# Sparse attention and a rational MLP on one core: another way in for the first two batches

## The reference

```
# 8 batches, 8 heads, 576 tokens, head size 64; q, k, v float32
scores = q @ k.T / 8
rel = pos[:, None] - pos[None, :]
mask_local   = (rel >= 0) & (rel < 32)                            # heads 0 to 3
mask_strided = (rel >= 0) & (pos[None, :] % 32 == pos[:, None] % 32)  # heads 4 to 7
attn = softmax(where(mask, scores, -1e9))
x = (attn @ v), heads side by side               # [4608, 512]
h = x @ w_in                                     # [4608, 2048]
P = a0 + a1*h + a2*h**2 + a3*h**3
Q = 1 + |b0|*|h| + |b1|*h**2
out = (P / (Q + 1e-6)) @ w_out                   # [4608, 512], float32
```

## Time and profile before

| | |
|---|---|
| median of 3 runs | 422.16 us (420.53 to 424.83) |
| the profiled execution | 421.72 us |
| its span, first to last instruction | 419.9 us |
| busy in the span: TensorE, VectorE, ScalarE | 330.4, 318.9, 323.1 us |
| DMA: moved, mean | 50.12 MB, 119 GB/s |
| share of the 16 DMA engines: q1 (SyncE's), q0 (POOL's) | 41.3%, 23.9% |

### The profile page before, as it was taken

How to read it: one execution, slowest core, us unless ns; L and a number is a source line. 1 busy time by engine, 2 the same in 40 slices (tenths; PEclk the granted TensorE clock), 3 DMA queues, 4 the chain that set the end, 5 groups by cost and what they waited for, 6 DMA issues and landing times.

```text
span 419.9 us, 10298 instructions
## 1 busy us (share of the span) xinstructions
PE 330.4 (79%) x4674; PEld 160.4 (38%) x4674; DVE 318.9 (76%) x266; ACT 323.1 (77%) x351; POOL 43.7 (10%) x70
## 2 busy tenths in 40 slices
PE   0104207979959998999799899999999999992995
PEld 0003105434424543444344444445444444440442
DVE  5002025488699769999589799988998998999992
ACT  0102015479897899999689899799999999999983
POOL 8000200204000050005006000230000000000000
PEclk9999999979988999999999999999999999997999
DMA  8999969958016959928988997499821000000232
GB/s 134 213 203 207 213 144 188 154 116 143 4 35 81 213 91 183 212 73 141 194 161 177 167 133 118 108 161 120 186 66 30 2 25 27 25 25 2 75 125 100
DMA packets 102899, 50.12 MB, mean 119 GB/s; under 512 B 90280, under 2 KB 95336, under 8 KB 102312
## 3 DMA queue, kind: packets, MB, share of 16 engines
q1 hardware_dynamic: 93576, 32.29, 41.3%
q0 software_dynamic: 9280, 17.18, 23.9%
HBM read 39.76 MB, written 19.46 MB: 141 GB/s over the span
## 4 chain that ended last, share of the span: by engine, by line
ACT 42%; PE 25%; DVE 11%; SPq 11%; DMA 7%; issue 4%; ACTq 0%
PE ps L833 12%; ACT z L784 10%; ACT u L798 9%; ACT h L768 9%; ACT u L803 9%; PE ps L764 8%; SPq L382 4%; SPq L392 4%; DVE u L794 4%; DMA out_dram<-os 3%; DMA ptL<-pL 2%; DVE u L791 2%; ACT os L841 2%; DMA z<-in_v_dram 2%; SPq L294 1%
## 5 line engine op out<-in xcount | busy, mean ns | idle before, releaser
L833 PE MATMUL ps<-Wout,h 128*128 128x512 bf16 x576 | 138.9, 387 | 8.6 <-DVE h L818 7.5
L764 PE MATMUL ps<-XT,Win 128*128 128x512 bf16 x576 | 137.6, 385 | 5.1 <-ACT h L768 2.6
L768 ACT ACTIVATE h<-ps 128x512 bf16<-128x512 f32 x144 | 84.0, 673 | 11.4 <-PE ps L764 10.9
L833 PEld LDWEIGHTS ps<-Wout,h 128*128 128x128 bf16 x576 | 54.6, 99 | 73.9 <-DVE h L818 8.4
L764 PEld LDWEIGHTS ps<-XT,Win 128*128 128x128 bf16 x576 | 54.2, 99 | 73.8 <-ACT h L768 8.2
L798 ACT ACTIVATE u<-u,consts 128x2048 bf16<-128x2048 bf16 (+1 forms) x40 | 74.2, 1903 | 4.8 <-DVE u L794 4.8
L803 ACT ACTIVATE u<-u 128x2048 bf16<-128x2048 bf16 (+1 forms) x40 | 72.1, 1817 | 0.1
L784 ACT ACTIVATE z<-h 128x2048 bf16<-128x2048 bf16 (+1 forms) x38 | 69.4, 1871 | 0.2
L818 DVE TENSOR_TENSOR h<-z,u 128x4096 bf16<-128x4096 bf16 (+2 forms) x21 | 41.6, 1980 | 2.4 <-ACT u L803 1.8
L794 DVE TENSOR_TENSOR u<-u,z 128x4096 bf16<-128x4096 bf16 (+2 forms) x21 | 41.6, 1982 | 0.4
L814 DVE TENSOR_TENSOR z<-z,h 128x4096 bf16<-128x4096 bf16 (+2 forms) x21 | 41.5, 1977 | 0.3
(11 more groups left out here) (79 smaller groups left out, 227.4 us busy)
## 6 DMA issues: line engine op xcount, KB each, us to landing
out_dram<-os SPq DMA_DIRECT2D x36, 256.0 KB, 2.5
qk<-in_k_dram POOLq DMA_DIRECT2D x14, 288.0 KB, 6.5
qk<-in_q_dram POOLq DMA_DIRECT2D x14, 288.0 KB, 7.7
Win<-in_moe_w_in_dram POOLq DMA_DIRECT2D x2, 1024.0 KB, 30.5
Wout<-in_moe_w_out_dram POOLq DMA_DIRECT2D x2, 1024.0 KB, 31.6
v<-in_v_dram POOLq DMA_DIRECT2D x6, 288.0 KB, 8.8
vL<-v SPq DMA_DIRECT2D x24, 72.0 KB, 3.7
vS<-in_v_dram POOLq DMA_DIRECT2D x24, 72.0 KB, 6.9
```

The costliest lines, as they stand in the source:

```text
L764: r = e.matmul(bank(ph, 0, CH), Win[:, kk, f * 128:(f + 1) * 128], XT[:, kk, c * CH:c * CH + CH], start=(kk == 0), stop=(kk == NK1 - 1))
L768: P.op("act", lambda e, f=f, ph=ph, h=h, f0=f0: e.activation(h.t[:, f - f0, :], bank(ph, 0, CH), AF.Copy), "ev512", ("hev", c, f), r=[ph], ...
L833: r = e.matmul(bank(po, 0, Fout), h.t[:, j, m * 128:(m + 1) * 128], Wout[:, kk, :], start=(kk == 0), stop=(kk == NF - 1))
```

## The change

- The constants go first in SyncE's queue, in the order IDN, MS, M0, each mask with a tile of its own (T_ms, T_m0); the masks' matmuls now also wait for the turned q and k that they go before.
- q and k of batches 0 and 1 are cast straight into SBUF, by pairs of heads (eight DMAs a batch, local heads first), and turned by TensorE. Batch 1's strided pairs are staged in Wout's second half, whose load waits for their turns.
- For these two batches the strided V is cast by POOL straight into vS, as for the others. The local V comes as float32, its own blocks only, by SyncE and, for half of batch 0, by ScalarE; both halves are cast by VectorE and ScalarE, and VectorE makes the copy one block up by two copies across partitions (vshift). Batch 1's loads wait for the last strided k of batch 0.
- Weights: Win's halves and Wout's first half stand between the casts of batches 0 and 1, Wout's second behind those of batch 2.
- Ln takes its bias as a number. The argument `dma=` changed its form; it tells the planner what a transfer costs and makes no instruction.
- `ORDER` and `AT` are new throughout.

```
-    NQK, NP = 1, 2
+    NQK, NP = 2, 2
...
-            for i, (nm, s_t, h0) in enumerate((("qs", q, HL), ("ks", k, HL), ("ql", q, 0), ("kl", k, 0))):
...
+            for i, (nm, s_t, h0) in enumerate((("ql", q, 0), ("kl", k, 0), ("qs", q, HL), ("ks", k, HL))):
+                for pair in range(2):
+                    if b != 1:
+                        ap = XT[0:72, i, NT - 2048 + 1024 * pair:NT - 1024 + 1024 * pair]
+                    elif i < 2:
+                        ap = XT[0:72, 2 * i + pair, 1536:2560]
+                    else:
+                        ap = Wout[0:72, 4 * i + 2 * pair:4 * i + 2 * pair + 2, :].rearrange("p h c -> p (h c)")
+                    t = Tile(f"sg{b}{nm}{pair}", ap.rearrange("p (h c) -> p h c", h=2))
+                    if b == 2:
+                        t.prev = stage[0, nm, pair].w + stage[0, nm, pair].r
+                    if b == 1 and i >= 2:
+                        T_wout[1].over.append(t)
+                    else:
+                        early.append(t)
+                    stage[b, nm, pair] = t
+                    P.op("pool", lambda e, t=t, s_t=s_t, h=h0 + 2 * pair: e.dma_start(
+                        t.t, bass.AP(tensor=s_t.tensor, offset=rows(s_t, b, h),
+                                     ap=[[8 * D, 72], [S * D, 2], [1, 8 * D]])),
+                        "issue", ("cast", b, nm), w=[t], dma=(144, 97), after=after)
...
-        if b < 2:
-            return st
-        bulk(b, "v", v, 0, vs, b * HS, T_v[b], after)
...
     def early_v(b, st):
 
+        vgate = [x for p in range(2) for x in stage[0, "ks", p].w]
...
+            for hh in range(2):
+                P.op("act" if b == 0 and hh else "sp", lambda e, hh=hh, pair=pair, t=t: e.dma_start(
+                    t.t[64 * hh + 32:64 * hh + 64, 0:NB * 64].rearrange("p (m d) -> p m d", d=64),
+                    bass.AP(tensor=v.tensor, offset=rows(v, b, 2 * pair + hh),
+                            ap=[[D, 32], [LB * D, NB], [1, D]])),
+                    "issue", ("vf", b, pair), w=[t], dma=(576, 21), after=vgate if b else ())
+            for hh in range(2):
+                e_ = ("dve", "act")[hh]
+                P.op(e_, evict(e_, lambda hh=hh, pair=pair: vl.t[64 * hh + 32:64 * hh + 64, pair, :, 0:64],
+                               lambda hh=hh, t=t: t.t[64 * hh + 32:64 * hh + 64, 0:NB * 64].rearrange(
+                                   "p (m d) -> p m d", d=64)), "cast1152", ("vcast", b, pair), r=[t], w=[vl])
+        own = list(vl.w)
+        for hh in range(2):
+            P.op("dve", lambda e, hh=hh: e.tensor_copy(
+                vl.t[64 * hh:64 * hh + 32, :, 1:NB, :], vl.t[64 * hh + 32:64 * hh + 64, :, 0:NB - 1, :]),
+                "cp2210", ("vshift", b), w=[vl], after=own)
 
...
-        P.op("pe", smask, "smask", ("smask", b), r=[T_c, T_id], w=[SS])
+        P.op("pe", smask, "smask", ("smask", b), r=[T_ms, T_id, sqk], w=[SS])
...
-        P.op("pe", lmask, "lmask", ("lmask", b), r=[T_c, T_id], w=[SL])
+        P.op("pe", lmask, "lmask", ("lmask", b), r=[T_m0, T_id, lqt, lkt], w=[SL])
...
-    for i in range(2):
-        weights(i, Wout[:, 8 * i:8 * i + 8, :], w_out[1024 * i:1024 * i + 1024, :], T_wout, "wout")
     sts[1] = casts(1)
     loads(0, sts[0])
+    weights(0, Wout[:, 0:8, :], w_out[0:1024, :], T_wout, "wout")
     nxt = 0
     for b in range(B):
         if b + 1 < B:
             loads(b + 1, sts[b + 1])
+        if b == 0:
+            weights(1, Wout[:, 8:16, :], w_out[1024:2048, :], T_wout, "wout")
...
-        "27 25 82 29 95 31 35 33 83 39 37 84 236 96-98 86 100 93 105 103 91 113 107 114 109 108 249 119 110 "
+        "39 41 43 45 47 106-109 49 51 53 111 93-95 116 114 97 124-125 104 102 66 128 130 118-121 70 68 72 147 "
```

More of the change, by code:

```diff
@@ L248, in graph @@
     T_wout = [Tile(f"wout{i}") for i in range(2)]
+    for t in T_win + T_wout:
+        t.over = []
     XT = sb("XT", [128, NK1, NT])
@@ L322, in bulk @@
             bass.AP(tensor=s_t.tensor, offset=rows(s_t, b, h0), ap=[[n, 16], [1, n]])),
-            "issue", ("cast", b, nm), w=[t], dma=1.5, after=after)
+            "issue", ("cast", b, nm), w=[t], dma=(16, 1380), after=after)
     stage = {}
@@ L354, in casts, with weights @@
                         ap=[[32 * D, NI], [S * D, HL], [1, 8 * D]])),
-                "issue", ("cast", b, "vS"), w=[vS], dma=0.45, after=after)
+                "issue", ("cast", b, "vS"), w=[vS], dma=(72, 97), after=after)
         return st
-    def weights(i, into, src, T, nm):
-        T[i].new()
+    def weights(i, into, src, T, nm, after=()):
+        T[i].new(*T[i].over)
         P.op("pool", lambda e: e.dma_start(into, src.rearrange("(a p) n -> p a n", p=128)), "issue", (nm, i),
-             w=[T[i]], dma=5.9)
+             w=[T[i]], dma=(512, 172), after=after)
@@ L373, in early_v @@
             t.new()
             host.over = [t]
-            fs.append(t)
-        for pair in range(2):
-            t = fs[pair]
-            P.op("dve", lambda e, t=t: e.memset(t.t[:, 0:64], 0.0), "tiny", ("vfz", b, pair), m=[t])
-            t.new()
-            for sh in range(2):
-                for hh in range(2):
-                    P.op("sp", lambda e, hh=hh, pair=pair, sh=sh, t=t: e.dma_start(
-                        t.t[64 * hh + 32 - 32 * sh:64 * hh + 64 - 32 * sh, 64 * sh:NB * 64].rearrange(
-                            "p (m d) -> p m d", d=64),
-                        bass.AP(tensor=v.tensor, offset=rows(v, b, 2 * pair + hh),
-                                ap=[[D, 32], [LB * D, NB - sh], [1, D]])),
-                        "issue", ("vf", b, pair), w=[t], dma=0.9)
@@ L388, in early_v @@
-        t = fs[2]
-        P.op("dve", lambda e, t=t: e.memset(t.t[:, 0:2048], 0.0), "mset", ("vfz", b, 2), m=[t])
-        t.new()
-        for bq in range(4):
-            P.op("sp", lambda e, bq=bq, t=t: e.dma_start(
-                t.t[32 * bq:32 * bq + NI, 0:2048].rearrange("p (h c) -> p h c", h=HL),
-                bass.AP(tensor=v.tensor, offset=rows(v, b, HL) + 8 * bq * D,
-                        ap=[[32 * D, NI], [S * D, HL], [1, 8 * D]])),
-                "issue", ("vfs", b), w=[t], dma=0.4)
@@ L444, in loads @@
                             ap=[[D, 32], [LB * D, NB], [1, D]])),
-                    "issue", ("load", b, "vl"), r=[T_v[b]], w=[own], dma=1.0)
+                    "issue", ("load", b, "vl"), r=[T_v[b]], w=[own], dma=(576, 16))
         for hh in range(2):
@@ L458, in turn_qk @@
         n = 0
-        for nm, dst in (("qs", sqk), ("ks", sqk), ("ql", lq), ("kl", lk)):
-            src = stage[b, nm]
+        for nm, dst in (("ql", lq), ("kl", lk), ("qs", sqk), ("ks", sqk)):
             for pair in range(2):
+                src = stage[b, nm, pair]
                 e_ = ("dve", "act")[pair]
```

89 lines of the change are left out of this document (32 added, 57 removed), and 103 rows, old and new, of the table ORDER.

## The result

| | before | after |
|---|---|---|
| median, us | 423.50 (420.53 to 425.10, 4 runs) | 375.84 (372.78 to 377.38, 4 runs) |
| ratio | 1 | 0.8873 [0.8793, 0.8953] |
| span of the profiled execution, us | 419.9 | 373.6 |
| first matmul of w1, us | 75.42 | 40.45 |
| from there to the end, us | 344.5 | 333.15 |

The time fell by 47.7 us, some 11%; 382 us was forecast, 365 to 398 the range. Inside that sum two terms were off, in opposite directions: the first part ended 8 us later than forecast (40.45 for 32), and the second was 15 us shorter (333.15 for 348.1).

The account below looks back on a forecast made before the run. Data was taken to bound the first part, compute (ScalarE and TensorE) the second. First w1 at 32 plus 348 made a 380 us span; 1.8 and 0.4 us more gave 382, range 365 to 398.

Parts of the forecast that it names:

- The bound: Whole kernel: up to 75.4 us it waits for data with DMA engines full; the other 344.5 us wait for compute.
- The landing: First part, batch 0's loads: the last k pair lands between 13 and 15.5 us, 14 taken.
- the upper value: Batch 0's loads: 15.5 us for q and k if POOL's, SyncE's and ScalarE's queues take three turns, V landing with them.
- So the last k pair lands ..., 3.3 us, so 17.3: Batch 0's attention: transposes, eviction, strided mask and scores take 3.3 us from last k pair to maximum, at 17.3.
- From the maximum to the first w1: End of first part: 14.6 us as before, plus shifts 1.6 and turns 1.8, less masks 1.7 and local maximum 1.35.
- The second part: From first w1 to the end: 344.5 us as before plus 3.6 of ScalarE's added work, 348.1; new order at nothing.
- priced at nothing: Ln's bias as a number: takes away one more thing to load, no time counted.
- the second part tightens: Rival, second part: the new order removes two DMA waits and ScalarE's idling, some 12 us, total 370; chance 0.11.
- V last: Rival, first part: ScalarE's and SyncE's loads share one queue, V holds the attention, w1 at 38, 388 us; chance 0.13.
- Batch 2 last: Rival: batch 2's casts stand behind 6.1 MB; with slower DMAs TensorE waits some 10 us, 392 us; chance 0.09.
- The clock: Rival, second part: TensorE at 1.2 GHz for part of its matmuls gives back some or all gain, 425 us; chance 0.05.
- the band of the forecast itself: Whole time: start moved by 43 us, second part as before and 4 us more, 372 to 391 us; chance 0.62.

Follow-up runs that it names:

- the first w1 at 35.70: Changed kernel with batch 1's three turns ahead of the first w1 put behind the first four groups of w1; 375.60 us, ratio 0.8903.
- the second of the V runs: Kernel before with batch 0's V ahead of batch 1's on SyncE's queue and batch 1's V casts behind batch 0's attention; 419.08 us, ratio 0.9906.

## Why the prediction was right, and where two terms were not

- **The bound.** "The first part waits for data, the second for compute": borne out. The gain is 35 us in front and 11 behind.
- **The landing.** The last k pair had landed by 15.44, when SyncE's load that waits for it was issued: inside the 13 to 15.5 given, above the 14 taken. The three queues that were the condition of the upper value are there, but not its three turns: ScalarE's queue had moved 1093 of its 1184 packets by 3.5 us, when POOL's had moved one, and the rest by 6.25. That the upper value came out is luck; what held the last pair beyond 14 us is not shown.
- **The step that was short: "So the last k pair lands ..., 3.3 us, so 17.3".** The maximum came at 21.05. On TensorE the local mask, scores and negation (1.03 + 1.24 + 1.14 = 3.4 us) stand ahead of the strided turns and scores, so that the chain ran through them and not from the last landing; and a fetch took 0.50.
- **From the maximum to the first w1** 14.95 us were forecast and 19.4 measured. 6.67 of these are program fetches (0.66 + 2.24 + 3.77), a wait that the sum did not have; without them the stretch was 12.7, 2 us under the forecast, which was not taken apart. In all: 32.3 + 3.75 + 6.67 - 2.2 = 40.5. The trace of before had shown such a stall: 3.3 us of "issue" stand in front of the strided scores in the very row used for their duration, hidden there behind the wait for V.
- **The second part.** 348.1 forecast; less 3.8 of ScalarE's work, most of it Ln ("priced at nothing"), and 11.15 of its idle time: 333.15. The rival "the second part tightens" was right on the waits and their size (11 for "some 12"), and it was given 0.11; its total, 370 us, stood on a first w1 at 32.
- **"V last", "Batch 2 last", the clock.** The first fell with one queue. The second did not come about, but holding transfers in front of batch 2's casts showed its price. The clock was 0.96 in the second part, beside 0.97. In the first it fell from 1.00 to 0.77, at no cost to the small matmuls: 16 turns took 0.69 us at 6.63, where 1.00 was granted, and at 28.62, where 0.50 was.
- **The sum as a sum.** That 375.84 us lies in the band of the forecast itself, 372 to 391, is in part luck: the first part took 8 us more than forecast, the second 15 less. First part and second part were added as if each stood alone. A run says otherwise: with the first w1 at 35.70 instead of 40.45 the second part took 338.20 us instead of 333.15. Some of the 8 us lost in front is therefore in the 15 won behind, the same time counted from a later mark; how much was not settled.

## What to carry to other kernels

Where DMA engines are full, count an engine's own program among the transfers: many small matmuls in a row stalled here at every 128th, and a row marked "issue" in the middle of an operation is the sign. Reordering a queue pays only if every engine's order goes with it and the small loads stay in front; what moved this kernel's start was fewer bytes ahead of the first use. An operand that can be a number should be one when its engine is the bound, and a gain at a mark inside the program is a gain only if what follows the mark was waiting for nothing else.

## What was not expected of the hardware

- TensorE's stalls come every 128 matmuls with their weight loads. With a DMA share of 1.25 in 28 to 40 us they last 2.24 and 3.77 us, with 0.16 they last 0.59 and 1.59. Behind 16 long matmuls of w1 none shows. The packets of the instruction queue are of 16 KB (0.61 MB in 37).
- Ln with a bias from a tile takes 2047 ns for 128 x 2048, with a number 1956, in two runs of the changed kernel that differ in nothing else; for 1024 wide 1154 and 1059. The difference, 91 and 95 ns, doesn't grow with the width.
- A load of a kilobyte issued into a full queue took 20.24 us to land (consts, issued at 35.77 in the second of the V runs).
